# An attention, a routed feed-forward and a second attention on one core: SP waits for four more scatters, and one piece of VectorE's work moves by four turns

## The reference

```python
# layer 1, per head h and token t
state = gamma[h] * state + outer(k[t], v[t]);   y[t] = q[t] @ state / sqrt(D)
# layer 2, per token: e is argmax(logits), or the previous token's e where local_gate >= 0.5
out[s] = p[e] * (relu(x[s] @ w1[e]) @ w2[e])
# layer 3, per expert e of 4
scores = (x @ wq[e]) @ (x @ wk[e]).T / sqrt(64), masked causally
a = softmax(scores);   ye = a @ (x @ wv[e]) @ wo[e]
out += weight(e, token) * ye        # zero unless e is among the token's best two
```

## Time and profile before

| | us |
|---|---|
| median of 3 runs | 417.92 (417.62 to 418.06) |
| the profiled execution | 417.62 |
| its span, from the first instruction to the last | 416.1 |
| TensorE busy | 403.3 (97%) |
| VectorE busy | 252.9 (61%) |
| ScalarE busy | 230.0 (55%) |
| GpSimd busy | 79.8 (19%) |

### The profile page before, as it was taken

One profiled execution on the slowest core, in us unless ns is written; L12 is line 12 of the kernel. 1 busy time (PEld: TensorE's weight loads), 2 busy tenths in 40 slices (PEclk: granted clock), 3 DMA queues, 4 the chain that ended last, 5 costly groups with the idle time before them and its releaser, 6 DMA issues.

```text
span 416.1 us, 9668 instructions
## 1 busy us (share of the span) xinstructions
PE 403.3 (97%) x3276; PEld 358.3 (86%) x3277; DVE 252.9 (61%) x501; ACT 230.0 (55%) x505; POOL 79.8 (19%) x101
## 2 busy tenths in 40 slices
PE   6999998999999999999999999999999999999996
PEld 5887886898989898989999898899877889988785
DVE  1677778897646557484746464546877432687750
ACT  4876786353636455464646363344766552476643
POOL 1012115110000101010000002710687200044330
PEclk9999999999999999999999999999999999999999
DMA  8968788697787767776767931724100040220004
GB/s 268 382 188 289 264 313 302 247 338 271 251 302 245 266 219 264 230 272 238 258 202 258 318 139 53 223 78 114 39 2 2 2 152 1 76 76 0 0 0 151
DMA packets 31992, 75.82 MB, mean 182 GB/s; under 512 B 3822, under 2 KB 4078, under 8 KB 31966
## 3 DMA queue, kind: packets, MB, share of 16 engines
q1 hardware_dynamic: 25422, 57.07, 40.2%
q0 software_dynamic: 4080, 14.16, 10.0%
q10 hardware_dynamic: 2464, 4.27, 2.8%
HBM read 56.41 MB, written 15.93 MB: 174 GB/s over the span
## 4 chain that ended last, share of the span: by engine, by line
PE 87%; DVE 6%; issue 3%; ACT 2%; DMA 1%; ACTq 0%; POOL 0%; DVEq 0%; POOLq 0%
PE bank L1427 7%; PE bank L1448 7%; PE bank L1447 7%; PE bank L1446 7%; PE bank L1432 7%; PE bank L1425 7%; PE bank L1558 5%; PE bank L1541 4%; PE bank L1521 3%; PE bank L1494 3%; PE bank L1493 3%; PE bank L1495 3%; PE bank L1525 3%; PE bank L1258 2%; PE bank L1305 2%
## 5 line engine op out<-in xcount | busy, mean ns | idle before, releaser
L1021 DVE TENSOR_TENSOR w2l<-raw,w2h 128x1024 fp32r<-128x1024 f32 x32 | 37.1, 1220 | 39.4 <-ACT w2h L663 37.7
L1425 PE MATMUL bank<-xh,w1h 128*128 128x240 f32 x256 | 57.7, 273 | 0.7 <-ACT w2h L663 0.7
L1427 PE MATMUL bank<-xl,w1h 128*128 128x240 f32 x256 | 57.6, 275 | 0.0
L663 ACT ACTIVATE w2h<-raw 128x1024 fp32r<-128x1024 f32 x32 | 31.6, 1049 | 46.1 <-PE bank L1448 45.6
L1446 PE MATMUL bank<-w2h,hh 128*128 128x512 f32 x128 | 50.6, 395 | 0.0
L591 POOL TENSOR_SCALAR att<-att,stat,mixw 128x128 f32<-128x128 f32 (+5 forms) x48 | 34.0, 715 | 84.2 <-DVE stat L1205 84.1
L1448 PE MATMUL bank<-w2h,hl 128*128 128x512 f32 x128 | 49.9, 390 | 0.0
L1447 PE MATMUL bank<-w2l,hh 128*128 128x512 f32 x128 | 49.9, 390 | 0.0
L1425 PEld LDWEIGHTS bank<-xh,w1h 128*128 128x128 f32 x256 | 48.7, 190 | 1.3 <-DVE xl L1027 1.1
L1427 PEld LDWEIGHTS bank<-xl,w1h 128*128 128x128 f32 x256 | 48.6, 190 | 0.3
L796 ACT ACTIVATE att<-bank,stat 128x128 f32<-128x128 f32 (+5 forms) x48 | 30.4, 633 | 13.3 <-DVE stat L1196 12.3
(11 more groups left out here) (186 smaller groups left out, 877.2 us busy)
## 6 DMA issues: line engine op xcount, KB each, us to landing
raw<-in_w SPq DMA_DIRECT2D x64, 512.0 KB, 5.3
xr<-tokens_by_expert POOLq DMA_DIRECT2D x8, 512.0 KB, 4.0
tokens_by_expert<-zero POOLq DMA_DIRECT2D x7, 512.0 KB, 4.9
kt_in<-in_kT SPq DMA_DIRECT2D x12, 256.0 KB, 5.1
q_in<-in_qT SPq DMA_DIRECT2D x12, 256.0 KB, 4.1
out<-osb SPq DMA_DIRECT2D x12, 256.0 KB, 2.0
v_in<-in_vR SPq DMA_DIRECT2D x11, 256.0 KB, 4.2
k_in<-in_kR SPq DMA_DIRECT2D x10, 256.0 KB, 5.1
```

The source lines that it names most:

```text
L663: act.activation(dst, source[:, q, :], ACT.Copy).then_inc(w_hi, 1)
L1021: dve.tensor_tensor(part(low), source[:, q, :], part(high).bitcast(F32), ALU.subtract).then_inc(w_lo, 1)
L1425: pe.matmul(to, w1h[:, dc, at], xh[:, dc, 0:TILE], start=(dc == 0 and fb % 2 == 0), stop=False, skip_group_check=True)
L1427: pe.matmul(to, w1h[:, dc, at], xl[:, dc, 0:TILE], start=False, stop=False, skip_group_check=True)
```

## The change

The low part of piece 7 is computed by VectorE at turn 5 instead of turn 9. SP waits for the scatters of the last four blocks (8 to 11) before it waits for the rows of the pads.

```diff
@@ -311,7 +311,7 @@
         QB_ORDER = (0, 1, 2, 3, 4, 5)
         EARLY = 1
         PROJECT_AT = (-1, -1, 1, 3)
-        LOW_AT = (-1, -1, 3, 9)
+        LOW_AT = (-1, -1, 3, 5)
         RECIP_AT, RECIP_FIRST = 2, 2
 
         def unit(n):
@@ -467,6 +467,8 @@
             for q in range(4):
                 sp.wait_ge(raw_in[q], 16)
                 load_w2(0, q, True)
+            for j in range(NB - HOT, NB):
+                sp.wait_ge(scattered[j], 16)
             sp.wait_ge(pads_ready, 1)
             for e in range(FIRST_PADS):
                 r = sp.value_load(pad_i[0:1, e:e + 1], min_val=0, max_val=E * REGION - TW)
```

## The result

The changed kernel took 424.18 us, the median of 4 runs (421.62 to 426.01), against 417.79 (417.62 to 418.06): a ratio of 1.0163, with a 95% interval of 1.0128 to 1.0198. It is slower, as forecast, but by 6.4 us and not by 2.4: outside the range. Two later comparisons in which the kernel before took 417.8 and 417.9 us gave the same, 425.04 and 424.46 us, ratios of 1.0154 and 1.0158. The changed kernel was measured beside the kernel before six times in all. The profiled execution of the first comparison took 426.06 us, with 424.5 us of span and a mean granted clock of 0.995. In this kernel and in the others with the four waits, lines behind L469 have numbers higher by 2.

A forecast was written before the change was run, and what follows sets the result against it. TensorE was taken to bound the span; 417.62 us plus 1.2 for the second tile plus 1.2 in the attention gave 420.0, stated as 420.2 for the median. The range was 418.3 to 421.6 us.

The forecast's parts named there:

- What bounds: Experts' stage: TensorE is busy for all 177.70 us, so a wait put there ends up in the time one for one.
- SP's reads move by 3.0 us: Before the pads: SP's first read moves from 72.6 to 75.6 us, and everything up to the second pad with it.
- TensorE stands for 1.3 us: Second token tile: load lands at 90.3 us, TensorE waits 1.3; taken as +1.2, bounds 0 to +2.6.
- The pad's time: Ahead of the tile load: the second pad lands 2.9 us after issue, at 81.4 instead of 78.4 us.
- There is no gain to be had: Second token tile: the change can win nothing there, because the tile is not late now.
- The load is slow because of SP's queue: Second tile's load: 8.1 us to land because w1 and zeros sit in SP's queue, against 4.1 unloaded.
- rival A: Second tile lands in time, within 6.9 us, only the attention cost stays: 419.1 us; chance 0.27 including D.
- Rival D: SP's added wait does nothing, scatters being in when VectorE has written the pads: 419.1 us; chance counted in A.
- Part 2: Attention: low half of q at VectorE's turn 5 delays TensorE, 0.5 us in first batch, 0.7 in second, +1.2 together.
- The stall before unit 12: Attention: TensorE's scores of unit 12 wait for the exponential of unit 10, 0.53 us once per batch.
- the 0.08 us that I had left to the gain: Attention: with no stall before unit 12, transposes of unit 8 start only 0.08 us earlier, behind ScalarE's copy of unit 7.
- Rivals B and C: B: little delay, tile wait hidden, within 0.8 us of 417.9, chance 0.14; C: stall gone, tile in time, 416.7, 0.06.

The follow-up runs named there:

- first comparison: The whole change against the kernel before, first measurement: 424.18 us against 417.79, ratio 1.0163.
- sixth comparison: The unchanged changed kernel measured again beside the kernel before: 424.46 us against 417.89, ratio 1.0158.
- fifth comparison: The unchanged changed kernel measured again beside the kernel before: 425.04 us against 417.80, ratio 1.0154.
- waits alone: Only SP's four waits added to the kernel before, low half left at turn 9; three comparisons: ratios 1.0057, 1.0041, 1.0045.
- ten traces of the table: Traces with the waits ahead of the pads and w1 queued behind: the changed kernel, SP's waits without the low half's move, w1 behind landed pads; ratios 1.0041 to 1.0163.
- the two with the quiet queue: SP also waits for the second tile's load before loading w1: with only the four waits added, ratio 0.9994; with the whole change, 1.0026.
- trace of turn 12: Kernel before with the low half of piece 7 at turn 12, scores of unit 12 waiting for piece 6 only: 417.96 us against 418.34, 0.9996.
- the parts alone: Each half of the change by itself against the kernel before: low half at turn 5, ratio 1.0032; SP's four waits, 1.0057, 1.0041 and 1.0045.
- changed kernel with the quiet queue: Changed kernel in which SP also waits for the second tile's load before loading w1, against the kernel before: 419.27 us against 418.34, 1.0026.
- third comparisons: The third comparison: the unchanged changed kernel measured again beside the kernel before, 426.41 us against 424.31, ratio 1.0062.
- waits already met: Kernel before plus four waits ahead of the pads, but on scatters of blocks 0 to 3, landed long before: 423.64 us against 423.44, 1.0006.
- waits with the quiet queue: Kernel before plus SP's four waits, and SP loads w1 only after the second tile's load has landed: 423.21 us against 423.39, 0.9994.

## Why the prediction was wrong

- **What bounds: right.** All that TensorE waited for in the experts' stage is in the end time.
- **SP's reads move by 3.0 us: right.** The pads go at 77.40 and 78.59 in the sixth comparison and at 77.82 and 79.01 in the fifth (forecast 77.2 and 78.5). In the other condition the kernel before issues them at 77.16 and 78.38 and the waits alone at 80.40 and 81.60: 3.2 us.
- **"TensorE stands for 1.3 us": this is the step that failed.** The chain was right, and its size in two traces of ten, but the other eight have 2.6 to 4.8 us. I gave every link one value, and for the bound varied only the load, the one that I thought doubtful: 2.6 us at most. In the fifth comparison the misses all go one way: the pads 0.5 us later than forecast, the second pad 4.6 us to landing and not the 2.9 of the earlier trace rows (1.7), the load 8.6 and not 8.1 (0.5), and TensorE at the tile 0.87 us earlier, since its experts start earlier. That is 3.6 us on top of 1.3, and 4.8 were measured. In the sixth it is 0.1, 0.9 and 0.5 us, and 2.8 measured.
- **The pad's time: the term that was mis-sized most.** I took the 2.9 us of the kernel before for the moved pad too; it took 3.0 to 4.6 us in the ten traces of the table, and 2.9 and 4.7 in the two with the quiet queue. It is not w1 right behind it (4.6 us without). The sixteenth of the pad's reports is what comes late. In two traces the pad's last packets wait behind 16 KB of the `instruction` queue, to which the delay of three microseconds moves the pad; for the 0.7 us of five others the cause stays open.
- **The clock: missing from the sum.** In the five traces with gaps of 1.2 to 2.8 us the gap costs itself; in the five with 3.0 to 4.8 us the clock falls to 0.50 and they cost 1.4 to 2.5 us on top. The kernel before has the clock at 1.00 all through its experts, and I did not name it as a bound.
- **"There is no gain to be had": wrong by 0.6 us.** The experts start 0.6 us earlier, by TensorE's shorter register reads. Where the tile is late this buys nothing, since TensorE then stands 0.6 us longer for it: it is 0.61 of the 0.87 us above.
- **The load is slow because of SP's queue, against rival A: right.** 8.2 to 9.3 us beside it, 4.1 and 4.2 with the queue quiet. Rival D (the wait does nothing) has fallen too.
- **Part 2: right in mechanism and size.** The stall before unit 12 was 0.58 us and not 0.53, as four transposes and the next scores are 0.36 us apart where I worked out 0.41; nothing rests on that. The early low half costs 0.6 us in batch 0 and 0.8 in batch 1 in every trace with it at turn 5 (forecast 0.5 and 0.7); unit 4 at 298.00 against 298.03, unit 8 at 304.75 against 304.67, behind the copy of unit 7. In the trace of turn 12 not even the 0.08 us that I had left to the gain appeared. Rivals B and C fall.

So the change costs 6.4 to 7.2 us where the kernel before takes 417.8: 1.4 in the attention and the other 5 to 6 at the second tile and in the slow clock behind it, where 1.2 was forecast. Where the kernel before takes 423 to 424 us it costs less, 1.0087 in the mean of three comparisons (3.7 us), and the parts alone, 1.0032 and in the mean 1.0048, add up to that. Why it costs less there is not settled; traces with tile parts of 4.4 and 7.0 us are among those.

## To carry over

Where a chain of several transfers ends with little slack before the engine that bounds, take every link at its worst value for the upper bound, not only the doubtful one, and add what the clock costs when that engine stands still for microseconds. A wait costs by what is queued behind its instruction: the same four waits were free behind the pads. And when a stall is to be removed, look for the next wait on the same engine first: here a copy took all of it. A transfer that is moved meets other company: look what else the queues carry at its new place.

## What the runs showed of the hardware

The kernel before has two times, 417.8 to 418.3 us and 423.3 to 424.3, and the same chip gave the one in two sets of comparisons and the other in a third, so it isn't the chip. The trace of the slower one shows where. TensorE's transposes and ScalarE's copy of their bank, first in the kernel before at 417.6, then the same two in the same kernel at 422.8, where everything stands 3.2 us later by then:

```profile
265.26 0.66 PE L1457 MATMUL bank<-cst,x 128*128 128x128 f32 x4
```
```profile
265.96 0.60 ACT L754 ACTIVATE x2h<-bank 128x512 fp32r<-128x512 f32 x1 [1.90 <-PE bank L1457]
```
```profile
268.45 0.66 PE L1457 MATMUL bank<-cst,x 128*128 128x128 f32 x4
```
```profile
271.46 0.60 ACT L754 ACTIVATE x2h<-bank 128x512 fp32r<-128x512 f32 x1 [4.22 <-PE bank L1457]
```

The copy starts 0.70 us after the transposes in the one and 3.01 in the other: TensorE's release reached ScalarE 2.3 us late, on an engine that was idle. The same happens in layer 1, at the blocks behind whose matmuls GpSimd issues pairs of indirect DMAs (at about 30, 40, 50 and 61 us), 0.5 to 2.2 us each, 3.0 us in all. In the trace at 417.6, and in those of the fifth and sixth comparisons and of the changed kernel with the quiet queue, no release is late like that. What makes it is not settled; that it is no property of the change is, since the unchanged kernel has it. In this condition the clock can fall elsewhere too: it is at 0.50 for 3.4 us, from a start between 68.5 and 70.1 us, in the traces of the first and third comparisons, of the waits already met and of the waits with the quiet queue. The kernel before has a mean clock of 0.996 or less in 4 of 23 to 12 of 18 of its executions there. That may be why the ratios spread more there.
